# A token mixer with three stages on one core: running totals of the first batch on TensorE, and four weight pieces split later

## The reference

```
# attention: a complex decay for each feature, S is 48x48 for each head
mag = sqrt(a_re^2 + a_im^2); scale = min(mag, 0.999) / (mag + 1e-6)
S_t = (a_t * scale_t) * S_{t-1} + k_t v_t^T ;  y_t = q_t . Re(S_t)
# first MLP
u = x + (U V applied over the tokens) ;  x = u + relu(u @ w_ch1) @ w_ch2     # 384 -> 1536 -> 384
# mixing by angles, then a channel MLP
theta = x @ w_theta ; y = w_tok_r @ (x cos theta) + w_tok_i @ (x sin theta)
u = x + y ; out = u + relu(u @ w_ch)
```

## Time and profile before

| what | value |
|---|---|
| median of 3 runs | 779.67 us (779.47 to 780.95) |
| the profiled execution | 780.54 us |
| its span, first to last instruction | 778.8 us |
| PE busy | 710.3 us, 91% |
| DVE, ACT, POOL busy | 65%, 54%, 28% |
| PE in the chain that ended last | 83% |
| DMA, mean | 94 GB/s |

### The profile page before, as it was taken

One profiled execution on the slowest core, in us unless ns is written; L12 is line 12 of the kernel. 1 busy time (PEld: TensorE's weight loads), 2 busy tenths in 40 slices (PEclk: granted clock), 3 DMA queues, 4 the chain that ended last, 5 costly groups with the idle time before them and its releaser, 6 DMA issues.

```text
span 778.8 us, 13125 instructions
## 1 busy us (share of the span) xinstructions
PE 710.3 (91%) x4944; PEld 683.4 (88%) x4944; DVE 503.9 (65%) x918; ACT 417.3 (54%) x913; POOL 220.8 (28%) x175
## 2 busy tenths in 40 slices
PE   0028999999999999999999999999999999999998
PEld 0027879999999979999999979999999879999998
DVE  6978858699458758597458747597448832224634
ACT  8875757665464636673464637674463621223531
POOL 0003582433430053222530053223440000113350
PEclk9998999999999999999999999999999999999999
DMA  9645540010246850010136950010136840000121
GB/s 325 201 110 144 146 176 5 1 42 1 61 120 192 218 203 21 1 42 0 61 104 193 235 203 21 0 42 1 42 103 183 227 144 37 1 1 1 42 61 61
DMA packets 42734, 73.45 MB, mean 94 GB/s; under 512 B 8784, under 2 KB 23376, under 8 KB 42672
## 3 DMA queue, kind: packets, MB, share of 16 engines
q1 hardware_dynamic: 42384, 72.23, 31.6%
q10 hardware_dynamic: 288, 0.39, 0.2%
HBM read 48.96 MB, written 4.72 MB: 69 GB/s over the span
## 4 chain that ended last, share of the span: by engine, by line
PE 83%; DVE 7%; ACT 4%; DMA 3%; issue 2%; SPq 1%; DVEq 0%; ACTq 0%
PE bank L1181 80%; DMA region<-qk 2%; PE bank L1351 1%; DVE stream L924 1%; PE bank L1262 1%; PE bank L1191 1%; PE bank L1221 1%; DMA region<-stream 1%; DVE logr L862 1%; DVE ST L954 1%; DVE qk L937 1%; DVE phasor L913 0%; DVE phasor L904 0%; SPq L333 0%; ACT scale L626 0%
## 5 line engine op out<-in xcount | busy, mean ns | idle before, releaser
L1181 PE MATMUL bank<-uT,w_sb 128*128 128x384 f32 x864 | 167.8, 342 | 0.0
L1181 PE MATMUL bank<-hT,w_sb 128*128 128x384 f32 x864 | 165.0, 337 | 0.0
L1181 PE MATMUL bank<-tok,z 128*128 128x384 f32 x864 | 158.7, 337 | 0.6 <-issue 0.2
L1181 PEld LDWEIGHTS bank<-uT,w_sb 128*128 128x128 f32 x864 | 153.1, 192 | 1.5 <-ACT uT L691 1.2
L1181 PEld LDWEIGHTS bank<-hT,w_sb 128*128 128x128 f32 x864 | 151.2, 188 | 0.3 <-DVE hT L1083 0.3
L1181 PEld LDWEIGHTS bank<-tok,z 128*128 128x128 f32 x864 | 149.3, 188 | 1.8 <-POOL tok L511 1.8
L1083 DVE SCALAR_TENSOR_TENSOR hT<-bank,hT 128x384 fp32r<-128x384 f32 x96 | 52.8, 550 | 72.0 <-ACT hT L683 71.7
L683 ACT ACTIVATE hT<-bank 128x384 fp32r<-128x384 f32 x96 | 46.5, 484 | 83.3 <-PE bank L1181 83.1
L511 POOL TENSOR_TENSOR tok<-tok_low,tok 128x768 fp32r<-128x768 f32 x20 | 38.1, 1907 | 86.8 <-ACT tok L713 86.8
L1191 PE MATMUL bank<-ident,stream 128*128 128x128 f32 x72 | 11.3, 297 | 48.6 <-DVE stream L937 48.6
L519 POOL TENSOR_TENSOR x_sb<-uT 128x384 f32<-128x384 f32 x24 | 25.1, 1074 | 102.2 <-DVE uT L1077 69.2
(11 more groups left out here) (147 smaller groups left out, 1310.7 us busy)
## 6 DMA issues: line engine op xcount, KB each, us to landing
stream<-in_qk SPq DMA_DIRECT2D x24, 384.0 KB, 3.8
tok_low<-in_w_tok SPq DMA_DIRECT2D x20, 384.0 KB, 3.5
stream<-in_a SPq DMA_DIRECT2D x19, 384.0 KB, 4.4
scale<-in_w_tok SPq DMA_DIRECT2D x16, 384.0 KB, 4.2
w_raw<-in_w SPq DMA_DIRECT2D x12, 384.0 KB, 7.6
region<-qk SPq DMA_DIRECT2D x16, 256.0 KB, 3.6
region<-stream SPq DMA_DIRECT2D x15, 256.0 KB, 3.1
stream<-in_v SPq DMA_DIRECT2D x16, 192.0 KB, 4.9
```

The costliest lines, as they stand in the source:

```text
L1181: return t.matmul(o, lhsT, rhs, start=start, stop=stop, is_transpose=turned)
```

## The change

For batch 0 alone, `a` is laid out with tokens on partitions: tile c is now chunk c, 128 tokens by 384 features. The running total of the log decays over a chunk is a matmul against a triangle of ones counted from the middle of the chunk (`from_mid`, made by `first_masks`), 6 matmuls a chunk in fp32 (`first_sums`); ACT takes all 384 columns of a chunk in one Exp of either sign straight from the result (`first_decays`) and keeps the decays of all six chunks (`first_scale`, in the room of logr and phasor's neighbours). The running total of the turns is likewise matmuls (`first_turns`): 6 within the chunk and, from chunk 1 on, 3 more that add the reduced phase at the end of the chunk before. DVE reduces each (`first_phase`). The squares of the real part, its absolute value (folded in a sign) and the quotient are on DVE. Of the table loads in the preparation one remains, and the 1/pi scaling goes into `tri_turn`.

Of the weights, w1's pieces are ordered by halves of the hidden features; ACT rounds one piece in the preparation, seven in chunks 0 to 4, and four (numbers 8 to 11) in blocks n = 0, 2, 4 and 5 of the first MLP; POOL takes their rests between `squares` and `quotients` of batch 1. The unchanged DVE list of the MLP is as described above. SP now issues V ahead of the pieces, and the last stage's three pieces after the copies and gains of chunks 0 and 1 instead of ahead of them.

```diff
@@ sync
-            for n in range(PIECES, STAGED):
+            for n in range(4, 2 * PIECES):
                 load_piece(n)
             to_rows(0, 0)
             load_qk(0, 2)
             to_rows(0, 1)
             gains_to_rows(0)
+            for n in range(2 * PIECES, STAGED):
+                load_piece(n)
@@ gpsimd
+                    if b == 1 and c == 1:
+                        split(EARLY + 3)
...
-                for n in range(2 * PIECES - 2):
-                    if b == 0:
+                if b == 0:
+                    for n in range(EARLY):
                         split(n)
                 if not last:
                     for c in range(3):
                         squares(b_next, c)
-                if b == 0:
-                    split(2 * PIECES - 2)
-                    split(2 * PIECES - 1)
+                        if b == 0:
+                            split(EARLY + c)
                 for n in range(KD):
                     full_u(b, n)
                 if not last:
@@ scalar
+            def first_logs(c):
+                act.wait_ge(s_m2.sem, c + 1)
+                a.activation(ln_m2, ln_m2, ACT.Ln).then_inc(s_ln.sem, 1)
+                if c + 1 < C:
+                    first_square(c + 1)
...
+                a.activation(den, ln_m2, ACT.Exp, scale=0.5).then_inc(s_mag.sem, 1)
+                a.activation(cor, ln_m2, ACT.Exp, scale=-0.5, bias=ln_eps[:, :]).then_inc(s_eps.sem, 1)
...
+                a.activation(cor, cor, ACT.Ln, bias=1.0).then_inc(s_cor.sem, 1)
+                act.wait_ge(s_den.sem, c + 1)
+                a.activation(den, den, ACT.Ln).then_inc(s_lnden.sem, 1)
+                if c >= 1:
+                    first_decays(c - 1)
...
+                a.activation(den, den, ACT.Exp, scale=-1.0).then_inc(s_rden.sem, 1)
...
+            def first_sin_cos(c):
+                act.wait_ge(s_frac.sem, c + 1)
+                a.activation(cos, sin, ACT.Abs).then_inc(s_wrap.sem, 1)
...
+                a.activation(cos, cos, ACT.Sin, scale=-SIN_TURN, bias=half_pi[:, :])
+                if c + 1 < C:
+                    act.wait_ge(s_phase.sem, c + 2)
+                a.activation(sin, sin, ACT.Sin, scale=SIN_TURN).then_inc(s_phasor.sem, 1)
...
                 for c in range(C):
                     attention(b, c)
-                    if b == 0:
-                        round_piece(2 * c)
+                    if b == 0 and c < 2:
                         round_piece(2 * c + 1)
+                        round_piece(2 * c + 2)
+                    elif b == 0 and c < 5:
+                        round_piece(c + 3)
...
+                    if b == 0 and n in (0, 2, 4, 5):
+                        round_piece(EARLY + (n + 1) // 2)
...
+            first_square(0)
             for c in range(C):
+                first_logs(c)
+            round_piece(0)
+            first_decays(C - 1)
+            gains(0)
             nc.scalar.preload_act_table_set("trig_and_small")
             for c in range(C):
+                first_angle(c)
             for c in range(C):
                 if c == G:
-                    nc.scalar.preload_act_table_set("natural_log_exp_and_others")
-                    decays(0, 0)
-                    decays(0, 1)
-                    decays(0, 2)
                     first_rows()
-                    gains(0)
                     keys_to_sbuf(0, 0)
-                    decays(0, 3)
-                    nc.scalar.preload_act_table_set("trig_and_small")
-                if c + 1 < C:
-                    sin_cos(0, c)
+                first_sin_cos(c)
@@ vector
+            first_masks()
+            first_square_sum(0)
+            for c in range(C):
+                first_tangent(c)
                 if c >= 2:
+                    first_marks(c - 2)
+            first_marks(C - 2)
+            split_v()
+            first_marks(C - 1)
+            first_spans()
+            scaled(0, 0)
+            scaled(0, 1)
+            first_phase(0)
+            first_phase(1)
+            turned(0, 0, 0)
+            turned(0, 0, 1)
+            first_phase(2)
+            turned(0, 1, 0)
+            turned(0, 1, 1)
+            first_phase(3)
+            first_phase(4)
...
                     mask_scores(b, c, 1)
+                    if b == c == 0:
+                        first_phase(C - 1)
                     if c + 2 < C:
                         queries_keys(b, c + 2)
                     if c + 1 < C:
                         next_state(b, c)
-                    if b == c == 0:
-                        sum_turns(0, C - 1)
-                        reduce_phase(0, C - 1)
@@ tensor
+            def first_turns(c):
+                pe.wait_ge(s_atan.sem, c + 1)
+                for i in range(G):
+                    to, at = turns_bank[c][:, i * P:(i + 1) * P], slice(i * P, (i + 1) * P)
+                    mm(to, phasor[:, c, 1, at], tri_turn[:, :], start=i == 0, stop=False)
+                    ins = mm(to, phasor[:, c, 0, at], tri[:, :], start=False, stop=c == 0 and i == G - 1)
+                if c >= 1:
+                    pe.wait_ge(s_frac.sem, c)
+                    for i in range(G):
+                        last = phasor[:, c - 1, 1, (i + 1) * P - 1:(i + 1) * P]
+                        ins = mm(turns_bank[c][:, i * P:(i + 1) * P], ident[:, :], last.broadcast_to([P, P]), start=False,
+                                 stop=i == G - 1)
+                ins.then_inc(s_phase.sem, 1)
...
+            for c in range(C):
+                first_sums(c)
+            for c in range(G + 1):
+                first_turns(c)
             key_columns(0, 0)
+            first_turns(G + 1)
```

More of the change, by code:

```diff
@@ L437, in _ @@
             load_qk(0, 1)
-            for n in range(PIECES):
+            for i in range(3):
+                sp.dma_start(V3_raw[i * R:(i + 1) * R, :], V).then_inc(s_w["V"].sem, 16)
+            for n in range(4):
                 load_piece(n)
@@ L442, in _ @@
             for i in range(3):
-                sp.dma_start(V3_raw[i * R:(i + 1) * R, :], V).then_inc(s_w["V"].sem, 16)
-            for i in range(3):
                 sp.dma_start(U3[:, :, i, :], U.rearrange("(c p) r -> p c r", p=P)).then_inc(s_w["U"].sem, 16)
-            for n in range(PIECES, STAGED):
+            for n in range(4, 2 * PIECES):
                 load_piece(n)
@@ new lines, in first_decays, with first_angle @@
+            def first_decays(c):
+                act.wait_ge(s_first_sum.sem, c + 1)
+                exponent = sums_bank[c % 3][:, 0:G * SUMS].rearrange("p (i x) -> p i x", x=SUMS)[:, :, 0:P]
+                for j, sign in enumerate((1.0, -1.0)):
+                    ins = a.activation(first_scale[:, j, first_span(c)].rearrange("p (i t) -> p i t", i=G), exponent,
+                                       ACT.Exp, scale=sign)
+                ins.then_inc(s_exp.sem, 1)
+            def first_angle(c):
+                act.wait_ge(s_tan.sem, c + 1)
+                angle_c = phasor[:, c, 1, :]
+                a.activation(angle_c, angle_c, ACT.Arctan, scale=-4.0).then_inc(s_atan.sem, 1)
@@ L658, in attention @@
                     keys_to_sbuf(b, c)
-                if 1 <= c < C - 2 and (b or c >= 2):
+                if b and 1 <= c < C - 2:
                     decays(b, c + 2)
@@ new lines, in first_tangent @@
+            def first_tangent(c):
+                mag, ahead = phasor[:, c, 1, :], x_sb[:, c, :]
+                dve.wait_ge(s_first_abs.sem, c + 1)
+                dve.wait_ge(s_mag.sem, c + 1)
+                d.scalar_tensor_tensor(mag, ahead, -4.0, mag, ALU.mult, ALU.add).then_inc(s_den.sem, 1)
+                if c + 1 < C:
+                    first_square_sum(c + 1)
+                dve.wait_ge(s_den.sem, c + 1)
+                d.tensor_scalar(ahead, logr[:, c, :], 0.5, math.log(0.999), ALU.mult, ALU.min).then_inc(s_lnr.sem, 1)
+                dve.wait_ge(s_rden.sem, c + 1)
+                d.tensor_tensor(mag, a_part(0, c, 1), mag, ALU.mult).then_inc(s_quot.sem, 1)
+                half_tangent(0, c)
@@ new lines, in first_marks, with first_spans @@
+            def first_marks(c):
+                dve.wait_ge(s_exp.sem, c + 1)
+                d.tensor_copy(marks[:, :, :, c].rearrange("p e i -> p i e"),
+                              sums_bank[c % 3][:, 0:G * SUMS].rearrange("p (i x) -> p i x", x=SUMS)[:, :, P:SUMS])\
+                    .then_inc(s_marks.sem, 1)
+            def first_spans():
+                dve.wait_ge(s_marks.sem, C)
+                d.tensor_tensor(gain[:, :, :], marks[:, 1, :, 0:C - 1], marks[:, 0, :, 1:C], ALU.add).then_inc(s_span.sem, 2)
@@ L893, in half_tangent, with first_phase @@
+            def first_phase(c):
+                phase, whole = phasor[:, c, 1, :], phasor[:, c, 0, :]
+                dve.wait_ge(s_phase.sem, c + 1)
+                d.tensor_scalar(whole, turns_bank[c][:, 0:D], MAGIC, MAGIC, ALU.add, ALU.subtract).then_inc(s_round.sem, 1)
+                dve.wait_ge(s_round.sem, c + 1)
```

(10 more changed lines are left out.)

140 lines of the change are left out of this document (84 added, 56 removed).

## The result

The changed kernel takes 797.01 us (median of 4 runs, 794.31 to 800.41) against 779.57 beside it (4 runs): 1.0227 times as long, 95% interval 1.0195 to 1.0259. It is slower by 17.4 us, where 779.2 had been forecast and the range ended at 783.0. The profiled execution took 794.31 us with a span of 792.6, 13.8 more than the 778.8 of before. Of the four runs after, the two longest have the lowest mean granted clock (800.41 and 798.92 us at 0.970 and 0.976; 794.31 and 795.11 at 0.978 and 0.983).

The account below looks back on a forecast made before the run. PE was taken as nearly full after the start, so elsewhere only its waits count. 780.54 less 9.1 (start) plus 8.6 (first MLP) gave 780.0 for the profiled execution, 0.9 above the median: forecast 779.2 us, range 775.4 to 783.0.

Parts of the forecast that it names:

- The preparation: Start of the kernel, up to the first angle: loop about as long as before, first angle at 35.6 us, 5 us later.
- The landing: Chunk 0's second copy, issued at 46.9: lands 4.1 us later, between 3.1 and 4.96, so scores at 51.0, 4.1 us earlier.
- The first two chunks: Attention from the first scores to the transposes of chunk 2: 14.6 us instead of 19.2, 4.6 us gained.
- The later chunks: Attention: POOL's splits still hold DVE's state product once a chunk; chunks 2 to 4 gain 0.2 us, chunk 5 another 0.2.
- The pause in `down(4)`: First MLP: PE stands 6.8 us for DVE's hT, as DVE waits for POOL's quotient queued behind three splits.
- The half clock behind it: First MLP, after PE's pause in `down(4)`: PE works at half clock, losing 1.8 us, chosen over 2.8.
- No second pause: First MLP after `down(4)`: the other engines have made up ground, so PE does not stand again.
- the rivals: Three alternatives: no PE stand in the MLP (770.1 us, 0.10), phase chain at half clock (784.2, 0.17), full clock throughout (775.6, 0.10).
- the second rival: Preparation: phase chain runs at half clock, costing 5 us more, so the start gains only 4.1; 784.2 us, chance 0.17.
- The first rival: First MLP: PE does not stand there, so the start's 9.1 us are kept; 770.1 us, chance 0.10.
- the MLP's loss of 8.6: First MLP with four late pieces: PE's 6.8 us pause plus 1.8 at half clock, 8.6 us lost, between 7.8 and 10.

## Why the prediction was wrong, step by step

**The preparation** was 0.6 us late at the first angle: `first_turns(0)` started at 36.19, where 35.6 had been worked out (the 35.61 below is the start of Arctan, for 35.1). `split_v` was held by POOL's rest for 2.01 us in place of 0.55, the upper bound of 1.4, not the half that I took. PE's half clock then lasted to 41.5, not 39.4, and stretched the chain that the sine of chunk 2 waits for. Both together put the issue of the second copy at 48.18 for 46.9, 1.3 us late. ACT and its queue in after:

```profile
34.32 1.28 ACT L882 ACT_TABLE_LOAD   x1
35.61 2.59 ACT L640 ACTIVATE phasor<-phasor 128x384 f32<-128x384 f32 x6
...
48.18 0.69 ACTq L658 DMA_DIRECT2D region<-stream  x1
```

**The landing** was the mis-sized term beside it: 53.54 - 48.18 = 5.4 us from the issue, where I took 4.1 between 3.1 and 4.96. It lies outside both rows. The reason that I gave for less than 4.96, that the loads ahead had been under way for long, was an argument and no row. Both together make the first scores 2.5 us late.

**The first two chunks** were a little better than their sum, 13.9 us for 14.6, since the clock was full at the first scores of this execution (2.05 us). In four of the variants with the changed start they took 3.67 to 3.79, in the other four 2.19 to 3.25.

**The later chunks** were the step that failed in kind: "POOL's splits still hold DVE's product for the state once in a chunk" was read off the kernel before and carried over. But what is held depends on where DVE stands when ACT's rounding releases POOL. The chunk before had the rests on the product of the state, 1.6 to 2.1 us, which PE could bear, and its turns in the clear. The changed start shifts the two lists against each other, and a rest falls on the turns of chunk 4 that stand ahead of the state and the next mask. PE then waits 1.74 us at 79.39 and works on at half clock. That is 2.8 us from the transposes of chunk 2 to `up(0)`: 34.1 us, where 31.3 were forecast (31.7 less 0.4). With 2.5 and less 0.7 it makes the 4.6 that `up(0)` is late.

The Trainium skill, SBUF — State Buffer, section SBUF: two separate sides, states that POOL and a DVE instruction with two inputs in SBUF, among others, take a shared pair of ports for whole instructions and that the loser is blocked until the end. The rows agree: the second turn ends 0.8 us after POOL's rest (77.60 and 76.78), which is about one turn's own length, and with no rests the same instructions take 1.83 together. Not every instruction is held: the two masks at 70.71, with one input from PE's bank, took their usual 1.27 us beside the rest that ran from 70.32, and the product behind them waited. By the rows the price of a rest beside DVE is up to its whole 1.83 us on an instruction that it can hold; I had priced it for `split_v`, but not asked the same of each chunk.

**The pause in `down(4)`** was right, in place, chain and nearly in size: 7.41 us for 6.8, put down to DVE's hT, DVE waiting for the quotient. These are the rows (POOL, then DVE):

```profile
118.99 1.83 POOL L534 TENSOR_TENSOR w_sb<-w_raw,w_sb 128x768 fp32r<-128x768 f32 x1 [2.99 <-ACT w_sb L873]
120.78 2.89 POOL L547 TENSOR_TENSOR x_sb<-uT 128x384 f32<-128x384 f32 x3
...
125.19 0.99 POOL L519 TENSOR_TENSOR phasor<-stream,phasor 128x384 f32<-128x384 f32 x1
```

```profile
126.22 1.16 DVE L1011 SCALAR_TENSOR_TENSOR phasor<-phasor 128x384 f32<-128x384 f32 x1 [9.36 <-POOL phasor L519]
127.31 0.55 DVE L1199 SCALAR_TENSOR_TENSOR hT<-bank,hT 128x384 fp32r<-128x384 f32 x1
```

The quotient ends at 126.18, 22.6 us after `hidden(0)` at 103.57; 22.4 had been worked out. The rate in the Trainium skill's GPSIMD Engine Reference, section 2.1 Instruction dispatch, from which I estimated 1.6 us a rest, is given there as a floor. The three rests in the chain stayed above it, at 1.83 to 1.85; the row's 1.86 was the right term. `half_tangent(0)` took 1.16 beside POOL's next squares, not 0.55, and that is the 0.6. The half clock behind it held to about 134 us (0.50 in the windows from 126 to 133) and cost 2.8 us, not 1.8: of the two values in the trace I took the smaller, from a stretch with a shorter wait ahead of it.

**"No second pause"** failed: 1.75 us at 150.10, before the first rows of the second half. I had followed only hT, and the second pause is of uT, also made by DVE. It belongs to the late pieces, since it is missing with all of them early; but with the quotients first in POOL's list it is still 1.96 us, so the late quotient alone does not explain it, and what does stays open. Pace, pause, half clock and second pause give 0.8 + 7.4 + 2.8 + 1.8 = 12.8; `up(0)` at full clock gives 1.3 back, and 11.7 were measured.

**The steady loss** of 7.2 us was in no part and no rival. I read the new tiles as room, and costed them at nothing without naming what moves when they are put in. This is the term that failed with the least ground.

In sum, as the profiled executions stand: forecast -9.1 + 8.6; measured -4.5 + 11.7 + 6.6 = 13.8, of which 0.8 of the pace lie within the 11.7. None of the rivals happened. The phase chain did run at half clock for one burst longer than taken, but the clock rose at 41.5, and of the second rival's 5 us no more than 0.8 was paid, the part of the late issue that `split_v` does not explain. The first rival's time has a slip: without the MLP's loss of 8.6 the forecast of 779.2 becomes 770.6, not 770.1.

## What to carry to other kernels

Where work is moved into a list that is taken in order, ask what stands behind it and who wants that first: the order of POOL's list alone was worth 9.8 us here, with no work changed. A stall that is read off a trace belongs to an alignment of two engines' lists; if the change shifts one against the other, price the stall anew on every instruction that it could meet, and look for a gap where the other engine is idle. And compare the addresses of PE's operands before and after any new tile, and the starts of successive blocks at full clock: the means in the page's groups are blurred by half clock (`uT,w_sb` reads 339 to 344 ns at the good distances and 341 to 346 at the others; only the last stage's stand apart, as `tc_sb,xs` with 335 to 336 against 338 to 339). Padding is a one-line remedy if it is the right amount: 480 bytes brought the whole pace back here, 32 a quarter of it.

## What the runs showed of the hardware

The pace of fp32r matmuls of 128 columns by 384, operands in SBUF, depends on the distance between the two operands' addresses: nine take 1.560 us, or 1.590 with 32 bytes more per partition, or 1.584 with 64, or again 1.560 with 2048. It is not seen as a wait or in the clock, only in the starts and, less clearly, in the group means.

After waits of 1.74 us (at 79.39) and 7.4 us (at 127.91) PE worked at half clock for about 3 and 6 us; after a wait of 1.75 us in the same execution, at 150.10, it did not. Behind the waits of 0.9 to 1.0 us just ahead of `up(0)`, and those of 3.2 to 3.7 us at the first scores of the changed start, it was at half clock in some executions and not in others: 5.1 to 5.3 or 6.1 to 6.8 us for 27 matmuls, 2.05 to 3.79 us for the 16 records of the scores. Differences of 1 to 3 us between kernels whose lists are alike up to there should be read with that in mind. What decides it, what the 2 us are that the kernel shifted as a whole loses at full pace, and why the first copies land 5.4 us after their issue rather than 4.96, stayed open.
